# Key sums beside the state products, quartered causal scores, an earlier sigmoid and a reordered start, in a recurrent attention layer with two MoE layers

## The reference

```python
def _attn_ref(r, k, v, w, u):          # r, k, v: (4, 8, 768, 48); w, u: (8, 48)
    for t in range(S):
        cur = einsum('bhd,bhe->bhde', u[None] * kt, vt)
        y[:, :, t] = einsum('bhd,bhde->bhe', rt, state + cur)
        state = w[None, :, :, None] * state + einsum('bhd,bhe->bhde', kt, vt)

x = y as (3072 tokens, 384)
x = (silu(x @ w_gate) * (x @ w_val)) @ w_out              # 384 -> 1536 -> 384, all tokens
out = one of 8 experts for each token: relu(x @ w1) @ w2, # 384 -> 1024 -> 384
      times softmax gate of the expert, times sigmoid of x @ w_output_gate
```

## Time and profile before

| | |
|---|---|
| runs | 875.5, 875.4, 878.33 us; median 875.5 |
| profiled execution | 873.72 us, of which the span from the first to the last instruction 871.9 us |
| PE busy | 845.8 us, 97% of the span |
| DVE, ACT, POOL busy | 559.2, 319.4, 172.9 us |
| blocks 0 to 5 | about 27 to 573 us |

### The profile page before, as it was taken

One profiled execution on the slowest core, in us unless ns is written; L12 is line 12 of the kernel. 1 busy time (PEld: TensorE's weight loads), 2 busy tenths in 40 slices (PEclk: granted clock), 3 DMA queues, 4 the chain that ended last, 5 costly groups with the idle time before them and its releaser, 6 DMA issues. The chain is left out here.

```text
span 871.9 us, 19225 instructions
## 1 busy us (share of the span) xinstructions
PE 845.8 (97%) x7523; PEld 736.5 (84%) x7523; DVE 559.2 (64%) x1131; ACT 319.4 (37%) x522; POOL 172.9 (20%) x139
## 2 busy tenths in 40 slices
PE   7799999999999999999999999999899999999995
PEld 5578887788878888788777878899899999999995
DVE  7667746673666456744564446459969777887770
ACT  3422331112211131113111221347458666677651
POOL 2223203250233213230322001003111101111010
PEclk9899999999999999999999999999999999999999
DMA  9235301131122102220101002537986679666700
GB/s 351 103 112 200 132 1 57 58 116 35 37 78 94 57 1 78 92 94 1 58 23 38 1 1 65 227 136 244 381 304 258 233 251 327 254 250 248 275 17 19
DMA packets 23711, 115.66 MB, mean 133 GB/s; under 512 B 3324, under 2 KB 9392, under 8 KB 18016
## 3 DMA queue, kind: packets, MB, share of 16 engines
q1 hardware_dynamic: 19408, 98.96, 31.4%
q0 software_dynamic: 3520, 9.87, 3.0%
q10 hardware_dynamic: 720, 5.90, 2.0%
HBM read 101.63 MB, written 14.16 MB: 133 GB/s over the span
## 5 line engine op out<-in xcount | busy, mean ns | idle before, releaser
L1594 PE MATMUL bank<-X1H,WH 128*128 128x512 f32 x432 | 169.8, 394 | 1.1 <-DVE X L978 0.8
L1594 PE MATMUL bank<-X1L,WH 128*128 128x512 f32 x432 | 169.0, 392 | 0.1
L1594 PE MATMUL bank<-X1H,WL 128*128 128x512 f32 x432 | 168.8, 392 | 0.0
L771 ACT ACTIVATE SG<-bank 128x512 f32<-128x512 f32 x72 | 43.1, 599 | 250.2 <-PE bank L1594 250.2
L1207 DVE TENSOR_TENSOR TT<-bank,SG 128x512 f32<-128x512 f32 x72 | 49.8, 691 | 125.1 <-ACT SG L771 124.5
L683 ACT ACTIVATE AH<-PP 128x512 fp32r<-128x512 f32 (+1 forms) x78 | 46.1, 598 | 159.7 <-DVE PP L1212 159.7
L1594 PEld LDWEIGHTS bank<-X1H,WH 128*128 128x128 f32 x432 | 81.7, 189 | 19.3 <-issue 2.1
L1594 PEld LDWEIGHTS bank<-X1H,WL 128*128 128x128 f32 x432 | 81.6, 189 | 17.6 <-DVE WL L1031 0.3
L1594 PEld LDWEIGHTS bank<-X1L,WH 128*128 128x128 f32 x432 | 81.6, 189 | 17.1 <-DVE X1L L1037 0.5
L1640 PE MATMUL bank<-AH,WH 128*128 128x512 f32 (+1 forms) x234 | 91.7, 392 | 0.0
L1215 DVE TENSOR_TENSOR AL<-PP,AH 128x512 fp32r<-128x512 f32 (+1 forms) x78 | 57.5, 743 | 50.9 <-ACT AH L683 50.9
(11 more groups left out here) (220 smaller groups left out, 1814.2 us busy)
## 6 DMA issues: line engine op xcount, KB each, us to landing
W_EVEN<-w SPq DMA_DIRECT2D x20, 1536.0 KB, 8.2
W_ODD<-w SPq DMA_DIRECT2D x18, 1536.0 KB, 8.3
RK_IN<-unit_rk SPq DMA_DIRECT2D x20, 736.0 KB, 4.5
V_IN<-unit_v SPq DMA_DIRECT2D x20, 448.0 KB, 3.3
STG<-w_dense ACTq DMA_DIRECT2D x5, 1152.0 KB, 5.5
XG_ODD<-store SPq DMA_DIRECT2D x9, 394.0 KB, 8.5
store<-PAD SPq DMA_DIRECT2D x8, 394.0 KB, 4.5
RK_START<-unit_rk SPq DMA_DIRECT2D x4, 512.0 KB, 6.2
```

Of the source, the lines that this page charges most:

```text
L771: nc.scalar.activation(SG[:, :], GATE_PS[:, :], ACT.Sigmoid).then_inc(sig_ready, 1)
L1594: last = mm(bank_[:, :], lhs[:, f, m, k * P:k * P + P], rhs[:, k, :], start=(x == 0), stop=(x == len(terms) - 1))
```

## The change

On PE, `key_sums` is called within `outputs`, directly behind the state products, so at the odd step, and the wait for `gate_free` moves there with it. Scores of units from chunk 1 on are made as two matmuls for a head: early keys (64) by all 128 queries, and late keys by late queries (64x64); the late-keys-by-early-queries quarter is left as it is in `AM`, where chunk 0 wrote zeros. `mask_scores` follows with two operations for a half in place of one. On DVE `own_key` moves to the odd step, `decay_state` is gone and `add_state` is four `scalar_tensor_tensor` operations (multiply and add) on 112x64 each; the state terms go to bank 5 in place of bank 7. Routing work moves from steps 1, 3, 5 to 2, 4, 6 in blocks 1 to 4. On POOL `scale_rk` comes behind `scale_k` and `scale_r`. On ACT `first_state(2)` and `(3)` come behind the first `SG` and `AH`, and the first `load_dense(1)` behind the first `SG`. At the start the load of the constants is queued behind the first unit's keys, and the 22 transposes of 128 columns become 7 matmuls of 384 columns.

```diff
-                self.c_banks, self.u = (bank[7], bank[0]), bank[7]
+                self.c_banks, self.u = (bank[7], bank[0]), bank[5][:, PAIRS * VW:2 * PAIRS * VW]
...
-            sp.dma_start(CST[:, C_ID:C_ALL], consts[:, C_ID:C_ALL]).then_inc(consts_loaded, 16)
...
                     sp.dma_start(u.rk[:, :], unit_rk[u.i, :, 0:I_KT]).then_inc(u.rk_sem, 16)
+                    if u is u0:
+                        sp.dma_start(CST[:, C_ID:C_ALL], consts[:, C_ID:C_ALL]).then_inc(consts_loaded, 16)
...
             def scale_unit(u):
-                scale_rk(u)
+                u.wait_rk(pool)
                 scale_k(u)
                 scale_r(u)
+                scale_rk(u)
                 if not u.last:
                     scale_kt(u)
...
-            for b in range(BATCH):
-                first_state(b)
+            first_state(0)
+            first_state(1)
...
-                if first:
-                    act.wait_ge(dense_low, 3)
-                    load_dense(1)
-                else:
+                if not first:
...
                     nc.scalar.activation(SG[:, :], GATE_PS[:, :], ACT.Sigmoid).then_inc(sig_ready, 1)
+                    if first and f == 0:
+                        act.wait_ge(dense_low, 3)
+                        load_dense(1)
...
                         if f == 0:
+                            first_state(2)
+                            first_state(3)
...
-                if x == 4:
+                if x == 5:
                     key_products(u0)
...
+                    if u.first:
+                        last = tt(u.am[:, half, :, :], made, strict, ALU.mult)
+                    else:
+                        tt(u.am[EARLIER, half, :, :], made[EARLIER, :, :], strict[EARLIER, :, :], ALU.mult)
+                        last = tt(u.am[LATER, half, :, LATER], made[LATER, :, LATER], strict[LATER, :, LATER], ALU.mult)
+                    last.then_inc(masked, 1)
...
-                tt(ST[:, u.b, :, :], u.u[0:PR, 0:PAIRS * VW].rearrange("p (j e) -> p j e", j=PAIRS), ST[:, u.b, :, :],
-                   ALU.add).then_inc(state_ready, 1)
+                for s in range(PAIRS):
+                    last = stt(out=ST[:, u.b, s, :], in0=ST[:, u.b, s, :], scalar=WPOW[:, s, 7:8], in1=u.u[0:PR, s * VW:s * VW + VW],
+                               op0=ALU.mult, op1=ALU.add)
+                last.then_inc(state_ready, 1)
 
             def finish_unit(u):
-                if not u.last:
-                    decay_state(u)
...
                         if f % 2 == 0:
-                            own_key(u)
                             mask_scores(u)
                         else:
+                            own_key(u)
                             finish_unit(u)
...
-                        if f == (2 if last else 3):
+                        if f == (2 if last else 4):
                             route(n)
-                        if f == (3 if last else 5):
+                        if f == (3 if last else 6):
                             positions(n)
...
+                            mm(to[EARLIER, :], w[:, EARLIER], r, start=True, stop=True)
+                            last = mm(to[LATER, LATER], w[:, LATER], r[:, LATER], start=True, stop=True)
...
                         opened.add(at)
+                    key_sums(u)
                 u.wait_v(pe)
...
-            for x in range(22):
-                nc.tensor.transpose(bank[2][:, 0:P], ident, ident)
+            for x in range(7):
+                mm(bank[2][:, 0:3 * P], ident, CST[:, C_ID:C_ID + 3 * P], start=True, stop=True)
...
                         if f % 2 == 0:
-                            pe.wait_ge(gate_free, q + 1)
-                            key_sums(u)
                             scores(u)
                         else:
+                            pe.wait_ge(gate_free, q + 1)
                             outputs(u)
```

More of the change, by code:

```diff
@@ L989, in mask_scores @@
                     dve.wait_ge(scores_ready, 2 * u.i + half + 1)
[L990 to L997, removed]
+                    made = u.scores[half][:, :].rearrange("p (j t) -> p j t", j=PAIRS)
+                    strict = mask.unsqueeze(1).broadcast_to([P, PAIRS, P])
+                    if u.first:
[4 more added lines that the diff above has]
+                    last.then_inc(masked, 1)
             def add_output(u):
-                dve.wait_ge(y_ready, u.i + 1)
                 dve.wait_ge(c_used, u.i + 1)
+                if u.first or u.last:
+                    dve.wait_ge(y_ready, u.i + 1)
+                else:
+                    dve.wait_ge(u_ready, u.i + 1)
                 if u.first:
@@ L1230, in dense_block @@
                     if not first:
-                        if f == 1:
+                        if f == (1 if last else 2):
                             copy_logits(n)
-                        if f == (2 if last else 3):
+                        if f == (2 if last else 4):
                             copy_turned_logits(n)
-                        if f == (3 if last else 5):
+                        if f == (3 if last else 6):
                             copy_ranks(n)
@@ L1456, in key_sums @@
                 pe.wait_ge(c_used, u.i)
[L1457 to L1460, removed]
                 pe.nop(nofuse=True)
@@ L1496, in scores @@
                         pe.wait_ge(kh_copied, BATCH)
+                    else:
+                        pe.wait_ge(state_ready, min(u.i, UNITS - BATCH) if isinstance(u.i, int) else u.i)
+                    pe.nop(nofuse=True)
                 for s in range(PAIRS):
@@ L1499, in scores @@
                         a = Head(PAIRS * x + s)
-                        last = mm(u.scores[x][:, a.keys], u.kw[a.rows, a.keys], u.rw[a.rows, a.keys], start=True, stop=True)
+                        to, w, r = u.scores[x][:, a.keys], u.kw[a.rows, a.keys], u.rw[a.rows, a.keys]
+                        if u.first:
+                            last = mm(to, w, r, start=True, stop=True)
+                        else:
+                            mm(to[EARLIER, :], w[:, EARLIER], r, start=True, stop=True)
+                            last = mm(to[LATER, LATER], w[:, LATER], r[:, LATER], start=True, stop=True)
                         if s == PAIRS - 1:
@@ L1705, in dense_block @@
                     need(pe, gate_free, q)
-                    if f == 2 and not first:
+                    if f == (2 if last else 3) and not first:
                         pe.wait_ge(logits_copied, n)
-                    if f == (3 if last else 4) and not first:
+                    if f == (3 if last else 5) and not first:
                         pe.wait_ge(logits_read, n)
-                    if f == (4 if last else 6) and not first:
+                    if f == (4 if last else 7) and not first:
                         pe.wait_ge(ranks_copied, n)
-                    if f % 2 == 1 and f // 2 < len(units):
-                        pe.wait_ge(gate_sums_used, units[f // 2].i + 1 - BATCH)
+                    if f and f % 2 == 0 and f // 2 <= len(units):
+                        pe.wait_ge(gate_sums_used, units[f // 2 - 1].i + 1 - BATCH)
                     up(GATE_PS, 0, f, n).then_inc(gate_ready, 1)
@@ L1716, in dense_block @@
                     up(VALUE_PS, 1, f, n).then_inc(value_ready, 1)
-                    if not first and f in (0, 1, 2, 3, 5):
+                    if not first:
                         if f == 0:
                             turn(n)
-                        if f == 1:
+                        if f == (1 if last else 2):
                             pe.wait_ge(gate_free, q + 1)
                             route_logits(n)
-                        if f == (2 if last else 3):
+                        if f == (2 if last else 4):
                             pe.wait_ge(gate_free, q + 1)
                             turn_logits(n)
-                        if f == (3 if last else 5):
+                        if f == (3 if last else 6):
                             pe.wait_ge(gate_free, q + 1)
```

17 lines of the change are left out of this document (8 added, 9 removed).

## The result

The changed kernel takes **901.2 us** (median of 4 runs, 900.01 to 902.8) against 875.45 for the kernel before beside it: ratio 1.0288, interval 1.0261 to 1.0316. Forecast were 876.3, in a range of 868 to 882. The profiled execution took 900.76 us, with a span of 898.5.

The account below looks back on a forecast made before the run. PE, busy 97% of the span, was taken as the bound. Terms +2.9 -6.1 -3.1 +3.9 +4.6 -1.4 sum to +0.8 us on the profiled 873.72; with 1.8 for the median, 876.3 us, range 868 to 882.

Parts of the forecast that it names:

- At nothing: Parts priced at zero: `own_key` and state operations at odd steps, POOL's later `RXK` and `KH`, later record sends, SP's unit loads.
- records sent a step later: POOL's sends of a block's routed records, moved one step later by the change; priced at nothing.
- The start: Kernel start: constants queued later and new dummy matmuls delay the first dense matmul from 26.94 to about 29.8, +2.9 us.
- rival R2: At the start: the later start is hidden by slack; 873.4 us, no change; chance 0.14.
- Steps 0 and 1: Block 0: the 3.2 us gap becomes one of 2.0 elsewhere, half clock is not earned, outputs start earlier: -6.1 us.
- rival R3: Block 0, step 1: the half clock comes back behind the 2.0 us gap, +4.6, 880.9 us, slower; chance 0.16.
- One unit: The other 19 units: key sums fall away (0.60), odd step gains 0.44; -0.16 us each, -3.1 in all.
- R4: Scores: early and late quarters run one behind the other, 8.6 us over 19 units, 884.9 us, slower; chance 0.07.
- New waits for `TT`: PE waits at odd steps: 1.3 us three times in block 0 (+3.9); 0.8 at step 5, 0.35 at step 7, blocks 1-4 (+4.6).
- R5: Even steps: DVE's `AL` goes ahead of POOL's `KW`, eleven waits each 0.4 shorter, -4.2, 872.1 us, no change; chance 0.08.
- R1: Odd steps: no new waits for `TT`, without the 8.5 us; 867.8 us, faster; chance 0.15.

Follow-up runs that it names:

- late_sends_old_start_shifted: Changed kernel with block sends waiting for step 7's outputs, the old start, and 6 tiny dummy matmuls (12 passes) behind the transpositions: 877.15 us, ratio 1.0028 to the kernel before.
- late_sends: Changed kernel plus one POOL wait, so a block's four record sends start only when step 7's outputs are done: 881.63 us, ratio 1.01 to the kernel before.
- sends_one_by_one: Changed kernel with each of a block's four sends waiting until the one before has landed: 883.1 us, ratio 1.0072 to the kernel before.

## Why the prediction was wrong

**The step that failed** is in "At nothing": "records sent a step later". I moved the sends from step 6 to step 7 in the sum and put them at nothing without a reason. Where they went is beside 128 small passes; where they came from there were 48, and 43 to 49 are what PE ran through before each stall. The term measured 20.3 us in four pieces, and some 2 in the clock behind. The profile of before could not have priced it, since its sends met no long run of small matmuls; but the row of sends beside step 6 was in its timeline, and the question what a moved DMA will stand beside was not asked.

**The start**, +2.9: PE's first `turn_keys` came at 12.68 (12.4 forecast). The constants landed at 5.66 (6.1 forecast), but eight of the 14 dummy passes ran 0.64 us apart and six 0.32, where the forecast had five and nine: the high clock came 4.9 us behind PE's start and not 3.3. At the state terms of u2 the loss was 3.5; the two pairs of runs with and without gave 2.7 and 3.8 in the traces. On the way the old start had stood for a while (2.65 us from 22.73 to 25.38, where the same two groups of the new one start 1.01 apart, at 26.31 and 27.32), slack that I had said not to see: at the first dense matmul (28.88 for 26.94) the loss was 1.9, so rival R2 was a part of the truth. In step 0 it grew again, by a wait of 1.7 us for `X1L` that was not in the sum. From `turn_keys(u0)` to the first outputs the old start took 4.81 us and the new one 4.70, so the clock was nearly alike behind transposes and behind matmuls. The rule of the Trainium skill (TensorE: Matmul & The Clock Gate, "Part 4: PE-mode transpose") that transposes don't count for the clock would have made the old one much slower there; this trace does not bear it out.

**Steps 0 and 1**, -6.1: -4.1. The gap at the outputs was 2.35 us (2.0 forecast), and the granted clock fell to 0.50 behind it, from 44.7 to 48.1. So rival R3, the half clock behind a gap of 2 us, took place, at 1.6 to 2 us and not 4.6. In the execution of late_sends_old_start_shifted the clock stayed at 1.00 behind a gap as long, and the same stretch took 17.7 us for 23.4, -5.7.

**One unit**, -0.16: the odd piece 2.53 for 2.06 (+0.47; forecast +0.44), the even one 1.03 for 1.69 (-0.66; forecast -0.60). Right, and R4 (quarters one behind the other) is out. (19 times the forecast -0.16 is -3.0; the sum has -3.1.)

**New waits for `TT`**, +8.5 without the one in step 1: 7.2. Those of block 0 were 1.39 to 1.47 (1.3 forecast) and those of step 5 0.6 to 0.8 (0.8 forecast); step 7 had none (1.4 forecast). `KW` was ahead of `AL` (55.91 and 56.16), so R5 is out. What I did not see is whose they are: I let the mask's four operations "cancel" with `own_key`. Taking the quarters away took 7.0 of the 9.6 us of waits away, for 1.2 us more on PE. R1, no new waits, is thus near what the change would have been without the quarters: 0.6 us of waits are left outside step 1.

**Not in the sum**: pauses of about 1.3 us at certain places of PE's program within a piece of 128 passes, put down to its fetches of instructions; one in the profiled execution of the changed kernel, two or three in others.

With the sends out of the way (late_sends) the change is 1.0% slower, where 0.1% was forecast: the start, the pauses in step 5 and the clock in step 1 make the difference. The sigmoid's place alone gives 6.5 us. All parts together without the quarters, the sends beside step 7 and the new start give 7.3, and the sigmoid's place is one of them, so nothing clear of noise is shown for the others.

## What to carry to other kernels

When an edit moves a step of one engine, look up what its DMAs will stand beside, on engines that share nothing with it by semaphores: here a row of three or four indirect DMAs on POOL was free beside dense matmuls and cost 2 to 5.5 us beside a run of 64 to 128 small passes. Time that PE spends in `issue`, with no releaser, inside a group of small matmuls is the sign to look for. And test the parts of a bundled change alone: here the new place of one engine's operation brought nearly all that the best version of the bundle brought, and the quarters saved 0.06 us a unit on the busiest engine and cost 0.9 us on the engine that it waits for.

## What the hardware showed that was not expected

- Small f32 passes stall beside a row of POOL's indirect DMAs: 43 to 49 passes run, then 4 to 6 come every 0.73 us until about the row's end. Two sends in a row did not do it, three did, but one send followed by a wait for its landing cost 0.4 to 0.6 us (sends_one_by_one). Dense matmuls beside such a row kept 0.23 us each. Why is open.
- Pieces of 128 passes were 0.8 to 1.7 us longer in some executions, by one pause 2.1 to 2.4 us in. It comes at the same pass of a step in every execution that has it, and 8 passes more ahead brought it 8 passes earlier; 24 instructions more moved the pauses to another step. A fetch of 16384 bytes starts 0.5 to 1.3 us into each of these pieces, and into clean ones too.
- At the end of 18 of the 20 pieces stalled by three or four sends, or behind it, the granted clock went to 0.50. Behind the gap of 1.9 to 2.4 us in step 1 it fell in ten profiled executions and stayed at 1.00 in three.
